# One inverse of a head's row sums, for all six query tiles, in place of two for three tiles each

## The chip, the cores and the metric

The kernel runs on one core of a Trainium2 chip. The metric is the device time of one execution in microseconds. The work is one program for five engines: TensorE (PE, with its weight loads PEld), VectorE (DVE), ScalarE (ACT), GpSimd (POOL) and SyncE (SP), which meet only through semaphores.

## What is computed

A masked attention, a mixture of experts with one expert per token, and a dense layer with a rational activation, one after the other. The change touches the attention alone:

```python
scores = scale * np.matmul(q, k.transpose(0, 1, 3, 2))
scores = np.where(mask, scores, -1000000000.0)     # mask: query and key have the same nearest centroid
scores = scores - np.max(scores, axis=-1, keepdims=True)
attn = np.exp(scores)
attn = attn / (np.sum(attn, axis=-1, keepdims=True) + 1e-09)
return np.matmul(attn, v)
```

There are 2 x 8 = 16 heads of 768 queries and keys, 64 wide. What is changed is how the divisor `sum + 1e-09` is inverted.

## The kernel before

A head has six tiles of 128 queries, in two groups of three. The heads run in `steps`, a routine that each engine has of its own, with six steps i = 0 to 5 a head; heads 0, 1 and 14, 15 are written out, heads 2 to 13 run in a hardware loop of two heads a turn. In step i, PE transposes the probabilities of tile i (L387) into two PSUM banks, computes the scores of tile i + 2 (L347, L348; in steps 4 and 5 these are tiles 0 and 1 of the next head), and does a piece of other work: products with the values (L362, L363), the transpose back of a group's outputs (`back`, L371), and the preparation of the next heads (L321, L329, L334). ACT splits the transposed probabilities (L675, tile PTH) and computes the exponentials of tile i + 1 (L644), whose sums it leaves in SM. DVE takes the rest of the split (L1023, PTL), in steps 0 and 1 the one-hot rows of the next head (L972 to L980), and the row maximum of tile i + 2 (L962). POOL makes the operands of the head after (L837, L852, L854), the split values (L864, L866) and the mask rows (L872, L875), and in eight of the heads one piece of a weight (L834).

The chain that closes a step is: maximum (DVE), exponential (ACT), transposes (PE), split (ACT, then DVE). PE may transpose tile i + 1 into a bank only when DVE has taken tile i out of it, and only when that tile's exponential is there.

`inverse_sums` (two DVE instructions, L989 and L991) makes the inverses of three row sums in RS, a tile of three columns; `normalise` (L997) multiplies a group's outputs in PSUM by them and writes them to XO, and PE may fill the output bank again (`values`, part 0, L359) only when that is done. In the order of DVE's instructions, the inverses of a head's first group are made at the end of step 4 and used at the start of the next head's step 0; those of its second group are made at the end of the next head's step 1 and used at the end of its step 2. Below, "the boundary" of a head is the stretch from the row maximum of its step 5 to the first split of the next head's step 0. Behind an odd head of the loop DVE's sequencer also goes through the loop's branch there (L1056).

Of the kernel before, what the change touches and what calls it, by code (L numbers as in the profile page):

```python
# [6 lines left out]
ALU = mybir.AluOpType  # L7
# [3 lines left out]
P = 128  # L11
B, H, S, D = 2, 8, 768, 64
C = 16
HEADS = B * H
HP = HEADS // 2
JT = S // P
# [10 lines left out]
GT = 3  # L27
HG = JT // GT
# [16 lines left out]
def needed(v):  # L45

    return not (isinstance(v, int) and v <= 0)


def program(nc, q, k, v, cent, emb, tau, w1, w2, w_in, w_out, coef_a, coef_b, cst, tokid, out, dbg=None):  # L50
# [4 lines left out]
    with ExitStack() as ctx:  # L55
# [3 lines left out]
        def sem(name):  # L59
            return ctx.enter_context(nc.semaphore(name))  # L60
# [31 lines left out]
        def esb(name, shape, dt=F32):  # L92
            return early.enter_context(nc.sbuf_tensor(name, shape, dt))
# [21 lines left out]
        OS = esb("OS", [P, GT * P])  # L115
        NM = esb("NM", [P, 2, JT])
        SM = esb("SM", [P, 2, JT])
        RS = esb("RS", [P, GT])
        AMX, AM2 = esb("AMX", [P, 2 * JT]), esb("AM2", [P, 2 * JT])
        AEQ = esb("AEQ", [P, 2 * JT, C])  # L120
        OH = esb("OH", [P, JT, P], BF16)
# [43 lines left out]
        max_done, exp_done, pth_done, ptl_done = (sem(n) for n in ("max_done", "exp_done", "pth_done", "ptl_done"))  # L165
        os_done, rs_done, xo_done = sem("os_done"), sem("rs_done"), sem("xo_done")
# [764 lines left out]
        def _(dve):  # L931
# [28 lines left out]
            def rowmax(g, par, i):  # L960
                dve.wait_ge(s_done, JT * g + i + 1)
                nc.vector.tensor_reduce(NM[:, par, i:i + 1], s_bank(i % 2), AX.X, ALU.max, negate=True).then_inc(max_done, 1)  # L962

            def one_hots(g, n):

                dots = prep[:, 0:2 * JT * C].rearrange("p (a c) -> p a c", c=C)
                wide = [P, 2 * JT, C]
                if n:
                    dve.wait_ge(arg_step, 4 * g + n)
                if n == 0:  # L970
                    dve.wait_ge(prep_pe, PREPS * g + 4)
                    nc.vector.tensor_reduce(AMX[:, :], dots, AX.X, ALU.max).then_inc(arg_step, 1)  # L972
                elif n == 1:
                    nc.vector.tensor_tensor(AEQ[:, :, :], dots, AMX[:, :].unsqueeze(2).to_broadcast(wide), ALU.is_ge).then_inc(arg_step, 1)
                elif n == 2:
                    nc.vector.tensor_tensor(AEQ[:, :, :], AEQ[:, :, :], desc16.unsqueeze(1).to_broadcast(wide), ALU.mult).then_inc(arg_step, 1)
                elif n == 3:
                    nc.vector.tensor_reduce(AM2[:, :], AEQ[:, :, :], AX.X, ALU.max).then_inc(arg_step, 1)
                else:
                    nc.vector.tensor_tensor(OH[:, :, 0:4 * C].rearrange("p j (w c) -> p j w c", w=2)[:, :, :, 0:C],  # L980
                                            AEQ[:, :, :].rearrange("p (j w) c -> p j w c", w=2),
                                            AM2[:, :].unsqueeze(2).to_broadcast(wide).rearrange("p (j w) c -> p j w c", w=2),
                                            ALU.is_equal).then_inc(onehot_done, 1)

            def inverse_sums(g, par, grp):

                y = HG * g + grp
                dve.wait_ge(exp_done, GT * (y + 1))
                nc.vector.tensor_scalar(RS[:, :], SM[:, par, GT * grp:GT * (grp + 1)], 1e-9, None, ALU.add).then_inc(rs_done, 1)  # L989
                dve.wait_ge(rs_done, 2 * y + 1)  # L990
                nc.vector.reciprocal(RS[:, :], RS[:, :]).then_inc(rs_done, 1)  # L991

            def normalise(g, grp):
                y = HG * g + grp
                dve.wait_ge(rs_done, 2 * y + 2)
                dve.wait_ge(back_done, y + 1)
                nc.vector.tensor_tensor(XO[:, bass.ds(JT * (g // H) + GT * grp, GT), bass.ds(D * (g % H), D)],  # L997
                                        obank[:, 0:GT * D].rearrange("p (j d) -> p j d", d=D),
                                        RS[:, :].unsqueeze(2).to_broadcast([P, GT, D]), ALU.mult).then_inc(xo_done, 1)

            def early_logits(t):
                dve.wait_ge(lg_done, t + 1)
                nc.vector.tensor_copy(LG0[:, t, :], prep[:, 0:E]).then_inc(lg0_done, 1)

            def low_piece(w, par, p):
                dve.wait_ge(w_high, 8 * w + p + 1)
                nc.vector.tensor_tensor(LOW[par][:, p, :], RAW[par][:, p, :], HIGH[par][:, p, :].bitcast(F32), ALU.subtract).then_inc(w_low, 1)  # L1007

            def steps(h0, start=False, end=False):
                for par in range(2):  # L1010
                    for i in range(JT):
                        h = h0 + par
                        n = JT * h + i
                        far = end and par == 1
                        before = not (start and par == 0)
                        if i == 0:
                            if before:
                                normalise(h - 1, 0)
                        for hf in range(2):

                            dve.wait_ge(pth_done, 2 * n + 1 + hf)
                            at = (i % GT) * P
                            nc.vector.tensor_tensor(PTL[i // GT][:, 3 * hf:3 * hf + 3, at:at + P],  # L1023
                                                    pt_bank[hf].rearrange("p (a q) -> p a q", a=3),
                                                    PTH[i // GT][:, 3 * hf:3 * hf + 3, at:at + P].bitcast(F32), ALU.subtract).then_inc(ptl_done, 1)
                            if far and i and hf == 0:
                                early_logits(i - 1)
                        if i < 2 and not far:
                            for m in ((0, 1), (2, 3, 4))[i]:
                                one_hots(h + 1, m)  # L1030
                        if i < 4:
                            rowmax(h, par, i + 2)
                        elif not far:
                            rowmax(h + 1, 1 - par, i - 4)
                        if before and i == 1:
                            inverse_sums(h - 1, 1 - par, 1)
                        if before and i == 2:
                            normalise(h - 1, 1)
                        if i == 4:
                            inverse_sums(h, par, 0)  # L1040
                        if end and par == 0 and i < 4:

                            low_piece(0, 0, i)
# [9 lines left out]
            dve.wait_ge(pro_pe, 2)  # L1053
            nc.vector.tensor_copy(eT[:, :, :], obank[:, 0:KD * E].rearrange("p (a b) -> p a b", a=KD)).then_inc(pro_dve, 1)
            steps(0, start=True)
            with dve.Fori(1, HP - 1) as pr:  # L1056
                steps(2 * pr)
            steps(HEADS - 2, end=True)
            normalise(HEADS - 1, 0)
            early_logits(JT - 1)  # L1060
            inverse_sums(HEADS - 1, 1, 1)
            normalise(HEADS - 1, 1)
            if dbg is not None:
                return
# [200 lines left out]
```

## Time and profile before

| | before |
|---|---|
| median of 3 runs | 836.32 us (833.25 to 838.16) |
| the profiled execution | 837.4 us, its span 835.5 us |
| PE, PEld, DVE, ACT, POOL busy | 93%, 86%, 73%, 55%, 42% of the span |
| attention | from about 20 to 306 us of the span |
| L989, L991, L997 | 32 instructions each |
| granted TensorE clock | 0.956 over the span, 1.00 in the heads of the loop |

The span is what the profiler saw between the first and the last instruction. A line of a timeline gives the start of an instruction and its duration in us, its engine, its line in the kernel, what it writes and reads, and in brackets how long the engine had been idle before it and who ended that. On DVE the recorded start of an instruction overlaps the end of the one before by some 0.08 us when the two follow one another without a gap. A line of `DVEq` is work of DVE's sequencer: arithmetic on registers for semaphore values and addresses, branches, and waits.

### The profile page before, as it was taken

What the parts mean: (1) busy time and instruction counts of PE and PEld (TensorE: products, weight loads), DVE (VectorE), ACT (ScalarE), POOL (GpSimd) and SP (SyncE); (2) the same over time, 40 slices, a digit from 0 to 9 for tenths busy, and PEclk for the clock granted to TensorE, in tenths of its full rate; (3) what the DMA queues carried; (4) which work ended last, traced back from release to release, by engine and by line L of the source; (5) the groups of instructions that cost most, each with busy time, mean ns of one, the idle gap of its engine ahead of it and who ended that gap; (6) DMA issues with size and microseconds to landing.
All of it is one profiled execution on the core that took longest, in us unless ns stands there. A gap on an engine that the chain in (4) does not pass through costs nothing.

```text
span 835.5 us, 15711 instructions
## 1 busy us (share of the span) xinstructions
PE 773.8 (93%) x5429; PEld 721.2 (86%) x5430; DVE 613.5 (73%) x986; ACT 458.5 (55%) x867; POOL 354.2 (42%) x334
## 2 busy tenths in 40 slices
PE   7999999999998993299999999989999999999996
PEld 4898999999997883199999999988989999999995
DVE  4688888888889736156666667679987787778773
ACT  4677777778777752011111111137777776766762
POOL 3666667665665003605324455543232232313232
PEclk9799999999999985599999999989999999999998
DMA  9311111111100024416655456650000000000000
GB/s 268 75 29 31 38 47 29 28 38 44 32 35 1 1 95 170 140 27 227 209 187 171 164 177 223 201 202 1 1 11 16 1 26 2 25 0 25 0 26 26
DMA packets 67908, 63.61 MB, mean 76 GB/s; under 512 B 30872, under 2 KB 53528, under 8 KB 67872
## 3 DMA queue, kind: packets, MB, share of 16 engines
q1 hardware_dynamic: 65024, 56.62, 21.5%
q0 software_dynamic: 1920, 6.30, 2.0%
q8 instruction: 20, 0.33, 0.2%
q10 hardware_dynamic: 928, 0.23, 0.1%
q14 instruction: 16, 0.13, 0.0%
HBM read 56.32 MB, written 6.82 MB: 76 GB/s over the span
## 4 chain that ended last, share of the span: by engine, by line
PE 51%; issue 23%; DVE 13%; POOL 8%; ACT 2%; DMA 1%; POOLq 0%; DVEq 0%; ACTq 0%
PE PS L519 8%; PE PS L520 8%; PE PS L521 8%; PE PS L387 6%; POOL HL L910 5%; PE PS L362 3%; PE PS L363 3%; PE PS L347 3%; PE PS L348 3%; PE PS L329 3%; DVE NM L962 2%; DVE PTL L1023 1%; DVE w_low L1007 1%; POOL out L919 1%; PE PS L371 1%
## 5 line engine op out<-in xcount | busy, mean ns | idle before, releaser
L519 PE MATMUL PS<-XH,w_high 128*128 128x256 f32 x640 | 183.5, 287 | 7.6 <-DVE XL L1190 3.6
L520 PE MATMUL PS<-XL,w_high 128*128 128x256 f32 x640 | 183.0, 286 | 0.0
L521 PE MATMUL PS<-XH,w_low 128*128 128x256 f32 x640 | 182.9, 286 | 0.0
L834 POOL TENSOR_SCALAR w_high<-w_raw 128x1024 fp32r<-128x1024 f32 x80 | 102.4, 1300 | 129.2 <-DMA w_raw<-in_moe_w 103.7
L910 POOL TENSOR_TENSOR HL<-U,HH 128x512 fp32r<-128x512 f32 x48 | 62.5, 1301 | 185.9 <-ACT HH L773 185.9
L519 PEld LDWEIGHTS PS<-XH,w_high 128*128 128x128 f32 x640 | 124.8, 195 | 10.5 <-issue 8.8
L1023 DVE TENSOR_TENSOR PTL<-PS,PTH 128x384 fp32r<-128x384 f32 x192 | 98.3, 551 | 40.4 <-ACT PTH L675 40.3
L520 PEld LDWEIGHTS PS<-XL,w_high 128*128 128x128 f32 x640 | 124.8, 195 | 1.7
L521 PEld LDWEIGHTS PS<-XH,w_low 128*128 128x128 f32 x640 | 124.7, 195 | 0.0
L1007 DVE TENSOR_TENSOR w_low<-w_raw,w_high 128x1024 fp32r<-128x1024 f32 x80 | 115.1, 1465 | 9.4 <-issue 9.4
L675 ACT ACTIVATE PTH<-PS 128x384 fp32r<-128x384 f32 x192 | 85.1, 490 | 47.9 <-PE PS L387 47.3
L962 DVE TENSOR_REDUCE NM<-PS 128x1 f32<-128x768 f32 x96 | 90.9, 947 | 3.9 <-PE PS L348 3.9
L387 PE MATMUL PS<-consts,PR 128*128 128x128 f32 x576 | 85.0, 283 | 8.5 <-DVE PTL L1023 7.2
L644 ACT ACTIVATE PR<-PS,NM 128x768 f32<-128x768 f32 x96 | 86.9, 905 | 5.5 <-DVE NM L962 5.5
L752 ACT ACTIVATE HH<-PS 128x512 fp32r<-128x512 f32 x32 | 19.1, 597 | 118.1 <-PE PS L521 118.1
L387 PEld LDWEIGHTS PS<-consts,PR 128*128 128x128 f32 x576 | 68.3, 147 | 16.9 <-DVE PTL L1023 7.6
L519 PE MATMUL PS<-w_high,HH 128*128 128x512 f32 x192 | 75.6, 394 | 3.3 <-POOL HL L910 1.7
L347 PE MATMUL PS<-B,A 128*128 128x512 f32 x192 | 74.7, 389 | 0.8 <-POOL A L875 0.8
L520 PE MATMUL PS<-w_low,HH 128*128 128x512 f32 x192 | 75.3, 392 | 0.0
L521 PE MATMUL PS<-w_high,HL 128*128 128x512 f32 x192 | 74.7, 389 | 0.0
L519 PE MATMUL PS<-HH,w_high 128*128 128x256 f32 x256 | 73.1, 286 | 0.0
L520 PE MATMUL PS<-HL,w_high 128*128 128x256 f32 x256 | 72.4, 283 | 0.0
(178 smaller groups left out, 1742.0 us busy)
## 6 DMA issues: line engine op xcount, KB each, us to landing
w_raw<-in_moe_w SPq DMA_DIRECT2D x64, 512.0 KB, 8.0
xs<-xs_dram SPq DMA_DIRECT2D x9, 513.0 KB, 3.6
w_raw<-in_moe_w_in SPq DMA_DIRECT2D x8, 512.0 KB, 8.1
w_raw<-in_moe_w_out SPq DMA_DIRECT2D x8, 512.0 KB, 7.2
QK<-in_q SPq DMA_DIRECT2D x16, 192.0 KB, 3.1
V<-in_v SPq DMA_DIRECT2D x16, 192.0 KB, 2.4
QK<-in_k SPq DMA_DIRECT2D x15, 192.0 KB, 3.2
xs_dram<-zeros SPq DMA_DIRECT2D x1, 513.0 KB, 4.0
```

Of the source, the lines that this page charges most:

```text
L347: nc.tensor.matmul(o[:, lo:hi], A1[par][:, cols], B1[par][:, lo:hi], start=True, stop=False)
L387: last = nc.tensor.transpose(pt_bank[hf][:, j * P:(j + 1) * P], PR[i % 2][:, c:c + P], ident)
L519: nc.tensor.matmul(o, wh, xh, start=first, stop=False)
L520: nc.tensor.matmul(o, wh, xl, start=False, stop=False)
L521: return nc.tensor.matmul(o, wl, xh, start=False, stop=last)
L644: nc.scalar.activation(PR[i % 2][:, :], s_bank(i % 2), ACT.Exp, bias=NM[:, par, i:i + 1], accum_out=SM[:, par, i:i + 1]).then_inc(exp_done, 1)
L675: nc.scalar.activation(PTH[grp][:, 3 * hf:3 * hf + 3, at:at + P], pt_bank[hf].rearrange("p (a q) -> p a q", a=3), ACT.Copy).then_inc(pth_d ...
L834: return nc.gpsimd.tensor_scalar(HIGH[par][:, p, :], RAW[par][:, p, :], 1.0, 0.0, ALU.mult, ALU.add)
L910: nc.gpsimd.tensor_tensor(HL[:, g:g + 2, :].rearrange("p a t -> p (a t)"), U[j % 2][:, :], HH[:, g:g + 2, :].rearrange("p a t -> p (a t)") ...
L962: nc.vector.tensor_reduce(NM[:, par, i:i + 1], s_bank(i % 2), AX.X, ALU.max, negate=True).then_inc(max_done, 1)
L1007: nc.vector.tensor_tensor(LOW[par][:, p, :], RAW[par][:, p, :], HIGH[par][:, p, :].bitcast(F32), ALU.subtract).then_inc(w_low, 1)
L1023: nc.vector.tensor_tensor(PTL[i // GT][:, 3 * hf:3 * hf + 3, at:at + P], pt_bank[hf].rearrange("p (a q) -> p a q", a=3), PTH[i // GT][:, 3 ...
```

## The change

RS gets six columns. `inverse_sums` works on all six sums of a head at once and stands at the end of step 5, in every head. It waits for the head's sixth exponential, and, from head 1 on, for the two `normalise` of the head before, since RS is written again. The two old calls (end of step 4, end of step 1 of the next head) and the one behind the last step are gone. `normalise` takes its three columns of RS and waits for the new count of `rs_done`. There are 16 pairs of L989 and L991 in place of 32.

```diff
-        RS = esb("RS", [P, GT])
+        RS = esb("RS", [P, JT])
...
-            def inverse_sums(g, par, grp):
-
-                y = HG * g + grp
-                dve.wait_ge(exp_done, GT * (y + 1))
-                nc.vector.tensor_scalar(RS[:, :], SM[:, par, GT * grp:GT * (grp + 1)], 1e-9, None, ALU.add).then_inc(rs_done, 1)
-                dve.wait_ge(rs_done, 2 * y + 1)
+            def inverse_sums(g, par):
+
+                dve.wait_ge(exp_done, JT * (g + 1))
+                if needed(g):
+
+                    dve.wait_ge(xo_done, HG * g)
+                nc.vector.tensor_scalar(RS[:, :], SM[:, par, :], 1e-9, None, ALU.add).then_inc(rs_done, 1)
+                dve.wait_ge(rs_done, 2 * g + 1)
                 nc.vector.reciprocal(RS[:, :], RS[:, :]).then_inc(rs_done, 1)
 
             def normalise(g, grp):
                 y = HG * g + grp
-                dve.wait_ge(rs_done, 2 * y + 2)
+                dve.wait_ge(rs_done, 2 * g + 2)
                 dve.wait_ge(back_done, y + 1)
...
-                                        RS[:, :].unsqueeze(2).to_broadcast([P, GT, D]), ALU.mult).then_inc(xo_done, 1)
+                                        RS[:, GT * grp:GT * (grp + 1)].unsqueeze(2).to_broadcast([P, GT, D]), ALU.mult).then_inc(xo_done, 1)
...
-                        if before and i == 1:
-                            inverse_sums(h - 1, 1 - par, 1)
                         if before and i == 2:
                             normalise(h - 1, 1)
-                        if i == 4:
-                            inverse_sums(h, par, 0)
+                        if i == 5:
+                            inverse_sums(h, par)
...
             early_logits(JT - 1)
-            inverse_sums(HEADS - 1, 1, 1)
             normalise(HEADS - 1, 1)
```

## Rows read from the trace of the kernel before

**Rows 1.** Busy time in one head: stretch and length, each engine's, then granted clock, DMA

```profile
116.19:133.00 16.81, 16.48 (x123) 15.35 (x122) 14.41 (x29) 13.11 (x30) 11.51 (x13) 1.00 0.15 35
```

**Rows 2.** Waits of PE's weight loads in 60 to 252 us: total, times, longest

```profile
PEld PS L387 <- DVE PTL L1023: 7.6, 23, 0.6
```

**Rows 3.** Chain of waits in one head, in order of time: start, length, what

```profile
115.54 0.62 DVE RS L989
...
116.30 0.57 DVE PTL L1023
```

**Rows 4.** All instructions of L989: duration in ns, least, median, most

```profile
L989 DVE TENSOR_SCALAR RS<-SM x32: 151/158/798, 38.7 to 305.1; 128x3 f32<-128x3 f32 x32
```

**Rows 5.** Timeline of POOL

```profile
29.32 0.51 POOL L864 TENSOR_SCALAR VS<-V 128x384 fp32r<-128x384 f32 x1
...
115.13 1.00 POOL L866 TENSOR_TENSOR VS<-V,VS 128x384 fp32r<-128x384 f32 x1
...
125.47 0.83 POOL L837 TENSOR_SCALAR A<-T 64x768 fp32r<-64x768 f32 x1
...
131.13 0.73 POOL L864 TENSOR_SCALAR VS<-V 128x384 fp32r<-128x384 f32 x1 [1.02 <-PE PS L363]
```

**Rows 6.** Timeline of DVE: the second pair of a head, and head 14's L989

```profile
115.46 0.70 DVE L989 TENSOR_SCALAR RS<-SM 128x3 f32<-128x3 f32 x1
116.19 0.18 DVE L991 RECIPROCAL RS<-RS 128x3 f32<-128x3 f32 x1
...
269.09 0.16 DVE L989 TENSOR_SCALAR RS<-SM 128x3 f32<-128x3 f32 x1
```

**Rows 7.** Timeline of DVE: two instructions that start together with one of POOL's

```profile
29.38 0.66 DVE L976 TENSOR_TENSOR AEQ<-AEQ,consts 128x192 f32<-128x192 f32 x1
...
131.13 0.36 DVE L980 TENSOR_TENSOR OH<-AEQ,AM 128x192 bf16<-128x192 f32 x1
```

**Rows 8.** Timeline of DVE: step 5 of head 5, the boundary, head 6

```profile
123.72 1.02 DVE L1023 TENSOR_TENSOR PTL<-PS,PTH 128x384 fp32r<-128x384 f32 x2 [0.64 <-ACT PTH L675]
124.66 0.95 DVE L962 TENSOR_REDUCE NM<-PS 128x1 f32<-128x768 f32 x1
125.53 0.35 DVE L997 TENSOR_TENSOR XO<-PS,RS 128x192 f32 x1
126.32 1.02 DVE L1023 TENSOR_TENSOR PTL<-PS,PTH 128x384 fp32r<-128x384 f32 x2 [0.45 <-ACT PTH L675]
127.43 0.36 DVE L972 TENSOR_REDUCE AMX<-PS 128x12 f32<-128x192 f32 x1
...
128.10 0.95 DVE L962 TENSOR_REDUCE NM<-PS 128x1 f32<-128x768 f32 x1
129.42 1.02 DVE L1023 TENSOR_TENSOR PTL<-PS,PTH 128x384 fp32r<-128x384 f32 x2 [0.37 <-ACT PTH L675]
...
301.31 0.36 DVE L997 TENSOR_TENSOR XO<-PS,RS 128x192 f32<-128x192 f32 x1 [0.16 <-PE PS L371]
```

**Rows 9.** Timeline of ACT: the last instruction of two exponentials

```profile
32.83 0.19 ACT L644 ACTIVATION_READ_ACCUMULATOR PR<-PS,NM 128x1 f32 x1
...
116.46 0.19 ACT L644 ACTIVATION_READ_ACCUMULATOR PR<-PS,NM 128x1 f32 x1
```

**Rows 10.** Timeline of PE's weight loads

```profile
33.68 0.19 PEld L347 LDWEIGHTS PS<-B,A 128*128 128x128 f32 x1
...
117.65 0.19 PEld L347 LDWEIGHTS PS<-B,A 128*128 128x128 f32 x1
...
127.20 0.19 PEld L362 LDWEIGHTS PS<-PTH,VS 128*128 128x128 f32 x1
...
301.78 0.19 PEld L362 LDWEIGHTS PS<-PTH,VS 128*128 128x128 f32 x1 [0.38 <-issue]
```

**Rows 11.** DVE's sequencer at the boundary of head 5: durations in ns, first and last start

```profile
L1056 DVEq ALU_OP  x1: 40/40/40, 124.2 to 124.2; - x1
...
L997 DVEq FUSED_REGOPS  x2: 46/154/263, 124.8 to 125.1; - x2
```

## The prediction

> **What bounds the kernel now.** I read the page first, then the attention alone, since nothing else is touched. Busy time in one head of the loop [rows 1]: the head takes 16.81 us and PE is busy for 16.48 of them at a granted clock of 1.00 (the 2.4 GHz level), so PE sets the pace and only its gaps can be won. The waits say which gaps [rows 2]: in eleven and a half heads, PE's weight loads waited 7.6 us in 23 waits, all for PTL, the split on DVE; that is two waits a head. The chain of waits places them [rows 3]: DVE's L989, 0.62 us of it on the path, then the split of step 2 at 116.30, whose end releases PE's transposes of step 3. So of a head's two pairs, the second one (end of step 1) lies on the path. The first (end of step 4) does not: DVE waits 0.64 us for ACT behind it, at 123.72 [rows 8].
>
> Why is one of the two long? L989 has a median of 158 ns and a maximum of 798 [rows 4]. The one of 0.70 us starts at 115.46 [rows 6] while POOL's L866 runs from 115.13 to 116.13 [rows 5], and ends at 116.16, 0.03 behind it; the other twelve of this kind are the same picture. In head 14, where POOL's instruction had ended, the same L989 takes 0.16 us [rows 6]. So it is held by a running POOL instruction. The Trainium skill, SBUF — State Buffer, "Who interferes with whom", says that the two engines share a port pair that a VectorE instruction of this kind needs for itself, that the one that issues first keeps it for its whole instruction, and that two-input instructions of VectorE are caught too; the trace agrees with all of it, here and in the two starts of [rows 7].
>
> **What the removal gives.** Without the pair at the end of step 1, the split of step 2 starts right behind the row maximum, 0.84 us earlier (116.30 less 115.46). That is not what PE gains: what is late next is tile 3's exponential, which ends at 116.46 + 0.19 = 116.65 [rows 9]. In head 0 such an exponential is the last to come: from its end, 32.83 + 0.19 = 33.02, to the weight load of L347 at 33.68 [rows 10] it is 0.66 us. Head 0 is written out; in the loop I add an estimated 0.06 for a register instruction behind the wait. So L347's load comes at 116.65 + 0.72 = 117.37 in place of 117.65 [rows 10]: **0.28 us a head**, for heads 1 to 13. The bounds are 0.34 (no register instruction) and 0.20 (twice that). In head 14 the pair is short, and 0.16 + 0.18 and its gaps less the overlap, 0.28, come off a path that ends in a split of the weights and PTL; gain 0.28. The first pair (step 4) stands before the 0.64 us of waiting, the one behind the last step before a wait for PE's `back`: nothing.
>
> **What the new place costs.** At the end of step 5 the new L989 starts 0.87 behind the row maximum's start, where L997 starts now: 125.53 [rows 8]. POOL is then in the fourth of its four L837, from 125.47 to 126.30 [rows 5]; this L837 starts 0.03 to 0.06 us before in all 14 heads that have it. Who gets the port? When both start within a hundredth (131.13 [rows 5, 7]), DVE goes first: L980 takes its usual 0.36, and L864 0.73 instead of 0.51. When POOL is 0.06 ahead (29.32 against 29.38 [rows 5, 7]), DVE is held: L976 ends at 30.04, 0.21 behind POOL's end, instead of taking 0.35. The 0.05 of the new place is nearer to the second row, so I take it that **the new L989 is held to 126.33**. The bounds are 0.16 us (won) and 0.80 (held). By the rule of the Trainium skill cited above, the first to issue keeps the pair, which would be L837, and the sum would be the forecast's; read as a rule on who starts moving data first, it would leave the tie open and allow rival 1.
>
> A second cost has no row. `normalise` comes right behind now. Today its sequencer work (address arithmetic, behind its wait for `rs_done`) runs while the row maximum is busy: two register instructions of 0.26 and 0.05 us, from 124.8 to 125.18 [rows 11]. With the wait for a reciprocal that has only just been issued, they come after it, in the open. Reciprocal 126.36 to 126.56 (0.18 for three columns [rows 6], 0.20 taken for six; at most twice 0.18). Then:
> - behind an even head: 0.03 for the semaphore, 0.34 for the register instructions, 0.05 to issue: L997 starts at 126.98 in place of 125.53, ends at 127.33.
> - behind an odd head the loop's branch stands there too. From L1056 at 124.2 to the end of L997's register work at 125.18 it is 0.98 us [rows 11], some 0.03 of it the issue of the row maximum; the 0.95 left starts when the reciprocal is issued (126.36): L997 starts at 127.36, ends at 127.71.
> - behind head 0 everything is written out and has no register work: L997 at 126.60.
>
> Lower bound of this cost: nothing, if the register work is ahead of the wait.
>
> PE needs L997 for L362, whose weights it loads at 127.20 [rows 10]. From L997's end to this load it is 0.11 in the one row where it is the last to come (301.31 + 0.36 to 301.78 [rows 8, 10]), and about 0.04 where the wait sits on the load itself, as behind odd heads. So PE is late by 127.33 + 0.11 - 127.20 = 0.24 (even) and 127.71 + 0.04 - 127.20 = 0.55 (odd); behind head 0 by nothing.
>
> DVE itself: two splits, 0.94 from start to what follows; L972 to the row maximum 0.67; row maximum to split 0.87 [rows 8]. Even: split at 127.25, L972 at 128.19, maximum at 128.86, split of step 1 at 129.73, and 1.71 on L980 at 131.44. Odd: the same 0.38 later, 131.82. POOL's L864 is released by PE: 131.13 + 0.24 = 131.37 (even), 131.13 + 0.55 = 131.68 (odd). So **the tie at 131.13 is broken**: POOL is ahead by 0.07 and 0.14. L980 is then held to L864's end plus 0.21: 131.88 + 0.21 = 132.09 and 132.19 + 0.21 = 132.40, in place of 131.49, late by 0.60 and 0.91. The maximum, the exponential and the transposes of step 3 hang on L980; the 0.28 comes off. Net: **0.32 slower a head behind an even one, 0.63 behind an odd one**.
>
> The added wait for `xo_done` is for a `normalise` three steps back; behind it on DVE stand L989, L991 and L997, and it costs one sequencer instruction, hidden behind the row maximum. The wait for the sixth exponential is met before step 5 (its transposes need it). No DMA is moved. The columns that L989 and the reciprocal have more are in the numbers above. In the last head, new L989, reciprocal and L997 follow one another with L997 waited for by PE (301.31 [rows 8]): 0.19 later.
>
> **The sum**, in the profiled execution: 6 even boundaries of the loop (behind heads 2 to 12) at +0.32 = +1.9; 6 odd (1 to 11) at +0.63 = +3.8; behind head 0 -0.28; head 14 -0.28; the last head +0.19. Together +5.3 us, 837.4 to 842.7. The profiled execution is 1.1 us over the median of the runs, so for the median 836.3 + 5.3 = **841.6 us**.
>
> **Rivals.**
> 1. *The port is won.* The new L989 is issued before POOL holds the pair and takes 0.16; L997 then starts at 126.33 (even) or 126.72 (odd), which the waits of DVE behind it cover (0.45 us before 126.32, 0.1 before 127.43, 0.37 before 129.42, and the overlaps of 0.08 [rows 8]; behind odd heads only just), and PE is not kept. Then only the gain is left: 13 x -0.28 - 0.28 + 0.19 = -3.8, 832.5 us. The same comes out if L989 is held but the register work runs ahead of the wait. For it: the threshold lies anywhere between 0.00 and 0.06, and behind head 1 the distance is only 0.03. Against it: the row at 0.06, and 0.05 is close to it. The Trainium skill, VectorE: DVE Perf Modes, "Rules for kernel authors", advises fewer instructions for chained ones ("Minimize op *count*, not sems"), and there are 32 fewer; that speaks for this side.
> 2. *Only the first tie is lost.* Behind even heads L980 is just 0.07 behind by a chain of five terms. If it still goes first, it is late by 131.80 - 131.49 = 0.31, which the 0.28 cancels: 6 x 0.03 + 3.8 - 0.37 = +3.6, 839.9 us.
> 3. *POOL's next instruction follows without letting DVE in*, L852 of 1.8 us: L997 would be late by 1.8 more and PE with it, 12 x 1.8 = 22 us more. Against it: L989 got in right behind L866 thirteen times although L834 was queued. That the change does not do what it says I see no way for.
>
> **How the numbers follow.** L989 held at most boundaries: 0.68, of which the forecast (841.6) has 0.42 and rival 2 (839.9) 0.26. Rival 1 (832.5): 0.28, some of it with a mixture over the heads. Rival 3: 0.02. The rest, 0.02, is what I have not seen. A measurement of this kernel can tell about 0.5%, 4.2 us, from no change: under 832.1 is faster, over 840.5 slower. The forecast lies over that line by 1.1 (0.8 of its chance), rival 2 under it by 0.6 (0.25 of its), rival 1 is 0.4 short of the other line (0.4 of its). That gives faster 0.12, within 0.5% 0.46, slower 0.42. The range has to take in rival 1 above and the bounds of the chain: 831.8 to 843.6. The forecast's own range is 839.5 to 843.6.
>
> **What would show it.** L989 x16, at the end of step 5, of about 0.8 us in 14 heads or 0.16; L980 of about 0.8 us or 0.36; PE's L362 of step 0 waiting for L997; PE's wait for PTL in step 3 gone in favour of the exponential; a head of the loop 17.3 us long on average, or 16.5. The forecast is wrong if L989 is short, or if L997 starts within 0.1 us of the reciprocal's end.

## The result and the profile after

The changed kernel takes 840.14 us (median of 20 runs, 836.51 to 843.66) against 834.23 us of the kernel before beside it (20 runs, 832.02 to 838.17). The ratio over the runs timed side by side is 1.0058, interval 1.0042 to 1.0074: 4.8 us slower, where the forecast had 5.3. (The two medians by themselves are 5.9 us apart; in what follows "ratio" is always the first kind.) 64 instructions of DVE became 32, and the kernel is slower.

Its profiled execution took 843.66 us. The page's span and busy times:

```profile
span 841.6 us, 15646 instructions
...
PE 775.0 (92%) x5429; PEld 722.5 (86%) x5430; DVE 612.5 (73%) x954; ACT 458.3 (54%) x867; POOL 349.8 (42%) x334
```

Two heads of the loop by windows, columns as in [rows 1]; the first contains the boundary behind an odd head (5), the second the one behind an even head (6):

```profile
116.10:133.60 17.50, 16.54 (x123) 15.43 (x122) 14.51 (x28) 13.09 (x31) 11.29 (x13) 1.00 0.13 34
133.60:150.74 17.14, 16.47 (x123) 15.44 (x122) 14.52 (x28) 13.03 (x31) 11.27 (x13) 1.00 0.14 34
```

PE has no more work than in [rows 1] (16.5 us at a clock of 1.00) and more idle time. Each window also carries what the one-hots' L980 costs at its start, not at its end (L980 runs from 115.84 and from 133.36, see below). The instructions of the new pair and of `normalise`, as in [rows 4]: duration in ns (least, median, most), first and last start:

```profile
L991 DVE TENSOR_SCALAR RS<-SM x16: 159/816/827, 41.7 to 305.8; 128x6 f32<-128x6 f32 x16
...
L993 DVE RECIPROCAL RS<-RS x16: 190/191/192, 42.6 to 306.0; 128x6 f32<-128x6 f32 x16
...
L999 DVE TENSOR_TENSOR XO<-PS,RS x32: 339/357/359, 42.8 to 310.7; 128x192 f32 x24, 128x192 f32<-128x192 f32 x8
```

L991 (L989 before) is now long in 14 of 16 cases; before it was in 13 of 32. The last normalisation, which ends attention, starts at 310.7; before it is at 305.8, 4.9 sooner; the other 1.4 of the 6.3 us between the two profiled executions lie behind attention. Of the 4.9, 0.7 had come up before the first head, where nothing is changed. The rows of ACT's L636, which comes once a head, show where the rest is. The first pair is of before, the second of after, each the third and the fifteenth of these instructions:

```profile
49.30 0.79 ACT L636 ACTIVATE OHT<-PS 48x768 f32<-48x768 bf16 x1
...
251.14 0.79 ACT L636 ACTIVATE OHT<-PS 48x768 f32<-48x768 bf16 x1
```

```profile
49.46 0.79 ACT L636 ACTIVATE OHT<-PS 48x768 f32<-48x768 bf16 x1
...
256.27 0.79 ACT L636 ACTIVATE OHT<-PS 48x768 f32<-48x768 bf16 x1
```

Between them lie the twelve boundaries behind heads 1 to 12: 201.84 us before and 206.81 after, +5.0. These **twelve heads** are the measure of the mechanism in what follows, since the start of the kernel, the first head and the stage behind attention differ between the profiled executions also where nothing was changed in them.

The waits in 60 to 252 us, the stretch of [rows 2]:

```profile
DVE XO L999 <- DVE RS L993: 7.2, 12, 0.8
PEld PS L387 <- DVE PTL L1025: 6.9, 11, 0.7
ACT PR L644 <- DVE NM L962: 5.6, 11, 0.6
PE PS L387 <- ACT PR L644: 5.4, 11, 0.6
PEld PS L362 <- DVE XO L999: 2.8, 6, 0.6
```

The 23 waits of [rows 2] are 11: the one that the held pair of step 1 caused is gone. In its place step 3 waits for the exponential (5.4 us), and PE waits for `normalise` (2.8), which waits for the reciprocal (7.2).

DVE's timeline at an even boundary (head 4) and at an odd one (head 5), to be laid beside [rows 8]:

```profile
109.09 0.95 DVE L962 TENSOR_REDUCE NM<-PS 128x1 f32<-128x768 f32 x1
109.96 0.81 DVE L991 TENSOR_SCALAR RS<-SM 128x6 f32<-128x6 f32 x1
110.81 0.19 DVE L993 RECIPROCAL RS<-RS 128x6 f32<-128x6 f32 x1
111.42 0.36 DVE L999 TENSOR_TENSOR XO<-PS,RS 128x192 f32 x1 [0.42 <-DVE RS L993]
...
115.84 0.70 DVE L980 TENSOR_TENSOR OH<-AEQ,AM 128x192 bf16<-128x192 f32 x1
...
126.24 0.95 DVE L962 TENSOR_REDUCE NM<-PS 128x1 f32<-128x768 f32 x1
127.10 0.81 DVE L991 TENSOR_SCALAR RS<-SM 128x6 f32<-128x6 f32 x1
127.94 0.19 DVE L993 RECIPROCAL RS<-RS 128x6 f32<-128x6 f32 x1
128.94 0.36 DVE L999 TENSOR_TENSOR XO<-PS,RS 128x192 f32 x1 [0.80 <-DVE RS L993]
...
133.36 0.67 DVE L980 TENSOR_TENSOR OH<-AEQ,AM 128x192 bf16<-128x192 f32 x1
...
150.48 0.36 DVE L980 TENSOR_TENSOR OH<-AEQ,AM 128x192 bf16<-128x192 f32 x1
```

And POOL's instructions that start beside them:

```profile
109.92 0.82 POOL L837 TENSOR_SCALAR A<-T 64x768 fp32r<-64x768 f32 x1
...
115.83 0.51 POOL L864 TENSOR_SCALAR VS<-V 128x384 fp32r<-128x384 f32 x1 [1.28 <-PE PS L363]
...
150.47 0.73 POOL L864 TENSOR_SCALAR VS<-V 128x384 fp32r<-128x384 f32 x1 [1.29 <-PE PS L363]
```

Three things are to be seen. L991 ends at 110.77, 0.03 behind POOL's L837 (110.74), as L989 did behind L866 in [rows 5, 6]. Behind the reciprocal DVE sits idle with nothing to wait for, 0.42 and 0.80 us: the register work of `normalise`. And L980, 0.36 us in [rows 7], takes 0.70 at 115.84 and 0.67 at 133.36. At 150.48 it takes 0.36 and POOL's L864 0.73: there DVE got the port.

### The profile page after: what moved, and what is told of

Read it like the earlier page. It is cut to its first block, busy times and chain, and to the rows that moved or that the text cites. A ratio compares the mean times of both kernels' runs of the same rounds, so it can differ in the third digit from the quotient of the medians.

```text
span 841.6 us, 15646 instructions
## 1 busy us (share of the span) xinstructions
PE 775.0 (92%) x5429; PEld 722.5 (86%) x5430; DVE 612.5 (73%) x954; ACT 458.3 (54%) x867; POOL 349.8 (42%) x334
## 4 chain that ended last, share of the span: by engine, by line
PE 44%; issue 26%; DVE 17%; POOL 8%; ACT 3%; DMA 1%; DVEq 1%; POOLq 0%; ACTq 0%
PE PS L519 8%; PE PS L520 8%; PE PS L521 8%; POOL HL L910 5%; PE PS L387 4%; DVE NM L962 4%; DVE PTL L1025 3%; PE PS L362 3%; PE PS L363 3%; PE PS L347 2%; PE PS L348 2%; DVE w_low L1009 1%; POOL out L919 1%; PE PS L321 1%; DVE RS L991 1%
## 5 line engine op out<-in xcount | busy, mean ns | idle before, releaser
L834 POOL TENSOR_SCALAR w_high<-w_raw 128x1024 fp32r<-128x1024 f32 x80 | 100.2, 1272 | 133.9 <-DMA w_raw<-in_moe_w 109.3
```

What stands on the lines that cost most here:

```text
L834: return nc.gpsimd.tensor_scalar(HIGH[par][:, p, :], RAW[par][:, p, :], 1.0, 0.0, ALU.mult, ALU.add)
```

## The experiments

All were timed beside the kernel before, in five rounds each. The twelve heads are from the profiled execution of each, in us against the 201.84 of the kernel before.

### The port alone: x1

```diff
+        RT = esb("RT", [P, 3, 4])
...
-                nc.vector.tensor_scalar(RS[:, :], SM[:, par, :], 1e-9, None, ALU.add).then_inc(rs_done, 1)
+                nc.vector.tensor_scalar(RT[:, :, 0:2], SM[:, par, :].rearrange("p (a b) -> p a b", b=2), 1e-9, None, ALU.add).then_inc(rs_done, 1)
                 dve.wait_ge(rs_done, 2 * g + 1)
-                nc.vector.reciprocal(RS[:, :], RS[:, :]).then_inc(rs_done, 1)
+                nc.vector.reciprocal(RS[:, :].rearrange("p (a b) -> p a b", b=2), RT[:, :, 0:2]).then_inc(rs_done, 1)
```

Everything is where the change has it; only the shape of the addition's output differs, so that its outermost size is 3 where the input's is 6.

> The changed kernel, but the sums plus 1e-9 go to a tile of three pairs set 4 columns apart (the reciprocal reads them there). Theory (POOL's running L837 holds the added instruction because it needs the port pair; the Trainium skill, VectorE: DVE Perf Modes, What auto-detection actually checks, says the two-port mode wants the outermost sizes of source and destination both even or equal, here 6 and 3): the instruction takes under 0.3 us in all heads, L997's successor starts about 0.6 earlier, PE is not kept, L980 keeps its 0.36; the gain of 0.28 a head is left: ratio to the kernel before about 0.995 (-3.8 us). Rival (the hold is something else, such as the wait for the exponential or the new wait for xo_done): it stays at 0.8 us and the ratio at 1.006.

Measured: 832.56 us against 835.91, ratio 0.9954 (0.9928 to 0.998); twelve heads -3.2. The forecast's rival 1 has -0.28 a head, 3.4 in twelve, and 832.5 us in all. One of the twelve heads is 16.89 us long in place of 16.53: there L980 (L981 here) lost its tie with POOL and took 0.67 us. So the tie is close even where `normalise` keeps nobody. The timeline of DVE and POOL at a boundary:

```profile
107.51 0.15 DVE L992 TENSOR_SCALAR RT<-SM 128x6 f32<-128x6 f32 x1
107.70 0.19 DVE L994 RECIPROCAL RS<-RT 128x6 f32<-128x6 f32 x1
108.31 0.36 DVE L1000 TENSOR_TENSOR XO<-PS,RS 128x192 f32 x1 [0.42 <-DVE RS L994]
...
107.48 0.83 POOL L838 TENSOR_SCALAR A<-T 64x768 fp32r<-64x768 f32 x1
```

The addition starts 0.03 behind POOL as before, and takes 0.15 beside it. The register work is in the open as ever (0.42), and costs nothing. The Trainium skill, VectorE: DVE Perf Modes, "What auto-detection actually checks", says that an operation with a single source, both source and output in SBUF, takes the mode that uses the second port if their outermost sizes are both even or equal; 6 and 3 are neither, and the trace agrees.

### The same detour with equal sizes: y1

To see that it is the sizes and not the other tile or the strides, `SM` was laid out as `[P, 2, 3, 4]` too, which makes them 3 and 3.

```diff
-        SM = esb("SM", [P, 2, JT])
+        SM = esb("SM", [P, 2, 3, 4])
...
-                nc.vector.tensor_scalar(RT[:, :, 0:2], SM[:, par, :].rearrange("p (a b) -> p a b", b=2), 1e-9, None, ALU.add).then_inc(rs_done, 1)
+                nc.vector.tensor_scalar(RT[:, :, 0:2], SM[:, par, :, 0:2], 1e-9, None, ALU.add).then_inc(rs_done, 1)
```

> The changed kernel with the sums plus 1e-9 in three pairs set 4 columns apart, as in x1_oneport, but now the sums themselves lie in three pairs set 4 apart too, so that outermost sizes of source and destination are equal (3 and 3). Theory (x1_oneport was not held because its sizes, 6 and 3, rule out the form that needs the port pair): the instruction is held again, 0.8 us in 14 heads, and the ratio is back at 1.004 to 1.007. Rival (the other tile or its address was what freed it in x1_oneport): under 0.2 us and 0.995.

Measured: 841.05, ratio 1.0053 (1.0029 to 1.0078); twelve heads +4.6. The addition is held again:

```profile
L992 DVE TENSOR_SCALAR RT<-SM x16: 159/816/832, 41.4 to 304.9; 128x6 f32<-128x6 f32 x16
```

### The pair ahead of the row maximum: x2

```diff
+                        if i == 5:
+                            inverse_sums(h, par)
                         if i < 4:
...
-                        if i == 5:
-                            inverse_sums(h, par)
```

> The changed kernel, but in step 5 the inverses stand ahead of the row maximum instead of behind it. Theory (half of the cost is the register work of the normalise, exposed because it follows the reciprocal at once): the added instruction is still held, now by the third L837, by up to 0.8 us, but the register work runs under the row maximum and the normalise follows it without a gap; PE is not kept, or by under 0.1 us, and L980 is not held: ratio 0.994 to 0.998. Rival (the 0.8 us of the hold alone sets the loss, wherever it stands in step 5): 1.004 to 1.006.

Measured: 833.65, ratio 0.9971 (0.9947 to 0.9996); twelve heads -3.3. DVE's timeline:

```profile
106.35 0.80 DVE L991 TENSOR_SCALAR RS<-SM 128x6 f32<-128x6 f32 x1
107.18 0.19 DVE L993 RECIPROCAL RS<-RS 128x6 f32<-128x6 f32 x1
107.29 0.95 DVE L962 TENSOR_REDUCE NM<-PS 128x1 f32<-128x768 f32 x1
108.15 0.35 DVE L999 TENSOR_TENSOR XO<-PS,RS 128x192 f32 x1
```

The addition is held as long as in the kernel after (0.80), by the L837 before, but a row maximum of 0.95 us covers the register work again: `normalise` starts 0.86 behind the maximum with no idle time. So the hold alone costs nothing at this place, and by x1 the register work alone costs nothing. Only the two in a row (0.65 and 0.4 to 0.8 us) outrun the waits of DVE that used to cover them.

### The one-hots' tie undone: x3

```diff
                 pool.wait_ge(v_in[par], 16 * (g // 2) + 16)
+                pool.wait_ge(onehot_done, g + 1)
```

This stands ahead of L864: POOL can't start there before L980 has ended.

> The changed kernel, but POOL's L864 waits for L980 (the one-hot rows) to be done, so it can't hold it. Theory (two steps of the loss: PE and the splits late by 0.3 to 0.7 us, then L980 held by L864): L980 takes 0.36 in all heads, behind even heads nothing is lost (+0.03), behind odd heads 0.4 remains: 6 x 0.03 + 6 x 0.41 - 0.4 = +2.3 us, ratio 1.003. Rival (L980's hold is hidden by what PE waits for anyway): 1.006 as without the wait.

Measured: 836.47, ratio 1.0000 (0.9974 to 1.0025); twelve heads +2.2, 2.8 less than in the kernel after. L980 is never held (357 to 359 ns in all), L991 still is. Windows of a head behind an even and one behind an odd head:

```profile
99.12:115.96 16.84, 16.46 (x123) 15.42 (x123) 14.23 (x29) 13.05 (x29) 11.33 (x12) 1.00 0.14 35
115.96:133.17 17.21, 16.55 (x123) 15.41 (x122) 14.20 (x29) 13.18 (x29) 11.32 (x12) 1.00 0.14 34
```

The heads are as long as expected (+0.02 behind even ones, +0.31 to +0.47 behind odd ones of the loop, where 0.03 and 0.41 were expected; only behind head 1 it is +0.11). The total is not: 1.003 was expected, which lies just outside the interval. In the profiled execution the difference lies outside the twelve heads: from the first L636 to the last normalisation, attention is 0.2 us longer than before, so the ends of it gain 2.0, where 0.4 was expected. Why they do was not taken apart. The kernel after gives the same price by itself: the two heads behind even ones in which its L980 took 0.36 us are 16.80 long, and the four in which it was held 17.14. A lost tie costs about 0.3 us of a head.

### The kernel before without the addition: x4

```diff
-                nc.vector.tensor_scalar(RS[:, :], SM[:, par, GT * grp:GT * (grp + 1)], 1e-9, None, ALU.add).then_inc(rs_done, 1)
-                dve.wait_ge(rs_done, 2 * y + 1)
-                nc.vector.reciprocal(RS[:, :], RS[:, :]).then_inc(rs_done, 1)
+                nc.vector.reciprocal(RS[:, :], SM[:, par, GT * grp:GT * (grp + 1)]).then_inc(rs_done, 1)
```

> The kernel before, at its old places with its two calls a head, but without L989: the reciprocal reads the sums directly. It leaves out the addition of 1e-9. Theory (all that the change could win was the hold of L989 at the end of step 1, and what is late next is the exponential): the gap of the split of step 2 closes by 0.65 to 0.7 us, PE gains 0.28 a head: 14 x 0.28 = 3.9 us, ratio 0.995. Rival (the count of instructions is what matters, not the hold): 32 instructions fewer of 0.16 us, of which half on the path, 2.5 us, ratio 0.997; rival (the whole hold is on the path): 13 x 0.62 = 8 us, ratio 0.990.

Measured: 831.06, ratio 0.9956 (0.9931 to 0.9981); twelve heads -2.9, most heads 16.53 us in place of 16.82. The second reciprocal of a head starts while L866 runs, and all 32 are short:

```profile
L989 DVE RECIPROCAL RS<-SM x32: 157/165/168, 38.9 to 301.6; 128x3 f32<-128x3 f32 x32
```

So the gain of 0.28 a head that the forecast gave the removal comes from this one addition; the reciprocal, which stays, costs nothing. The ratio alone couldn't tell this from the rival of 0.997, the lengths of the heads do; that it is the addition's hold and not the addition itself is shown by x8, which keeps it. In two heads L980 lost its tie (0.71 us), and these are 16.89 long. And a RECIPROCAL is not held where a TENSOR_SCALAR of the same shape is.

### The kernel before, L864 behind L980: x8

The edit of x3, made to the kernel before.

> The kernel before, only with L864 behind L980. L864 then starts about 0.55 us later and L866 within a few hundredths of the L989 of step 1. Theory (who starts first holds): if L866 is ahead, L989 lasts 1.0 us in place of 0.70, a head 17.1 us, ratio 1.005; if L989 is ahead or level, it takes 0.16, a head 16.5 us, ratio 0.995. Rival (the port has no part in it): L989 stays at 0.70 and the ratio at 1.000.

Measured: 830.59, ratio 0.9938 (0.9915 to 0.9962); twelve heads -3.6. The wait was put there for the order of the one-hots, and moved POOL's next one as well:

```profile
113.83 0.16 DVE L990 TENSOR_SCALAR RS<-SM 128x3 f32<-128x3 f32 x1
...
113.89 1.00 POOL L867 TENSOR_TENSOR VS<-V,VS 128x384 fp32r<-128x384 f32 x1
```

DVE starts 0.06 ahead of POOL and isn't held; POOL's instruction keeps its 1.00 us too. One wait on another engine gives all that the removal of a pair gives.

### A freer order, with the change and without: x5, x6, x7, y2

The runs so far leave PE a gap of 0.2 us a head (x1: busy for 16.34 of 16.54) and step 3 waiting for the split and the exponential. x5 has the change with the additions of x1, the place of x2, the wait of x3, and two moves in the order:

```diff
                         elif i == 2:
-                            if not far:
-                                prep_part(h + 1, 1 - par, 4)
                             if before:
                                 back(h - 1, 1)
+                            if not far:
+                                prep_part(h + 1, 1 - par, 4)
...
-                        if i < 2 and not far:
-                            for m in ((0, 1), (2, 3, 4))[i]:
+                        if i == 0 and not far:
+                            for m in (0, 1):
                                 one_hots(h + 1, m)
...
                             rowmax(h + 1, 1 - par, i - 4)
+                        if i == 1 and not far:
+                            for m in (2, 3, 4):
+                                one_hots(h + 1, m)
```

In step 1 the row maximum, on which an exponential hangs, goes ahead of the one-hots, and in step 2 PE does `back`, for which DVE waits, ahead of the one-hots' transposes.

> The changed kernel with all its collisions taken out and step 1 to 3 reordered: the sums plus 1e-9 in three pairs (no hold), inverses ahead of the row maximum in step 5, row maximum ahead of the one-hot rows in step 1, PE's transpose back ahead of the one-hot transposes in step 2, and L864 behind L980. Theory (what was late next behind the removed pair is the exponential of tile 3, so an earlier row maximum frees PE down to its own work): PE's transposes of step 3 follow the transpose back without a gap, a head of the loop 16.1 to 16.2 us in place of 16.82: 14 x 0.65 = 9 us, ratio 0.989 to 0.990. Rival (ACT becomes the bound, since the copy of the one-hot rows now stands late before its split): 16.4 to 16.5 us a head, ratio 0.994 to 0.995.

Measured: 823.30 us (822.34 to 825.85), ratio 0.9848 (0.9817 to 0.9878); twelve heads -7.0: the fastest version here, 1.5% under the kernel before. A head by windows, and PE's waits in 60 to 252 us:

```profile
110.67:126.85 16.18, 16.18 (x123) 15.24 (x121) 13.80 (x28) 12.89 (x30) 11.34 (x12) 1.00 0.15 36
...
PEld PS L388 <- issue: 1.3, 8, 0.2
```

PE is busy for the whole head at a clock of 1.00. The line of waits is the largest of PE's and of its weight loads; neither the split nor the exponential is among them. In the heads of the loop nothing is left to win from DVE. The heads are as expected (16.1 to 16.2 us), but the ratio is below the expected 0.989 to 0.990, and its interval leaves that out: in the profiled execution a shorter start and a shorter stage behind attention come on top, of which more below.

x6 is x5 without the wait ahead of L864.

> The same without L864 waiting for L980. Theory: the one-hot instructions stand one row maximum later and meet L864 and L866 of POOL, both are held, by some 0.4 and 0.5 us; the split of step 2 comes behind them: a head 16.5 to 16.6 us, ratio 0.995 to 0.997, so the order alone gives nothing over a free port. Rival (holds of the one-hot rows do not matter once the row maximum is ahead of them): as with the wait, 0.990.

Measured: 832.13, ratio 0.9944 (0.9922 to 0.9966); twelve heads -3.5. In DVE's and POOL's timelines two instructions of the one-hots are held in turn, one by each of POOL's:

```profile
113.42 0.64 DVE L977 TENSOR_TENSOR AEQ<-AEQ,consts 128x192 f32<-128x192 f32 x1
114.10 0.35 DVE L979 TENSOR_REDUCE AM<-AEQ 128x12 f32<-128x192 f32 x1
114.49 0.68 DVE L981 TENSOR_TENSOR OH<-AEQ,AM 128x192 bf16<-128x192 f32 x1
...
113.35 0.51 POOL L865 TENSOR_SCALAR VS<-V 128x384 fp32r<-128x384 f32 x1 [1.00 <-PE PS L364]
113.95 1.00 POOL L867 TENSOR_TENSOR VS<-V,VS 128x384 fp32r<-128x384 f32 x1
```

That one wait is worth half of what x5 gains in the twelve heads, and 8.8 us between the medians. An order on DVE is worth what POOL leaves of it.

x7 is the kernel before with x5's order and wait, and both old pairs.

> The kernel before with both its pairs of inverses at their old places, and only the reordering: row maximum ahead of the one-hot rows in step 1, transpose back ahead of the one-hot transposes in step 2, L864 behind L980. Theory: L989 of step 1 now starts some 0.2 us ahead of L864 and is not held (0.16 us); two short instructions on the path of 0.3 us are all that is left, 16.2 to 16.4 us a head, ratio 0.990 to 0.993, so most of the gain needs no change of the inverses. Rival (L989 is still held by POOL): over 16.7 us, ratio 0.998 or more.

Measured: 830.13, ratio 0.9925 (0.9895 to 0.9955); twelve heads -6.3, its additions never held (153/159/164 ns). So the new order and the wait together bring 6.3 of the 7.0 (the wait alone 3.6, x8), and the change, where no pair is held any more, 0.06 us a head. The medians of x5 and x7 are 6.8 us apart all the same, from six runs each. The profiled executions, the fastest of each, are 4.6 apart; 1.4 of that lie before the first head and 1.1 in the first (its L636 starts at 14.59 in x5 and 15.94 in x7, the next one at 30.33 and 32.75); what makes the start shorter I haven't taken apart, and it isn't put down to the change.

y2 is x5 with the plain additions of the change.

> As x5_free_slot, but with the plain inverses of the changed kernel (same tile, no pairs), ahead of the row maximum in step 5. Theory: the first instruction is held there for up to 0.8 us by an L837 as in x2_ahead, and since the normalise behind it has its register work under the row maximum, nothing of it reaches PE: 16.2 us a head, ratio 0.985 to 0.989, as x5_free_slot. Rival (with PE's slack gone the hold shows): 16.4 us a head or more, 0.990 or more.

Measured: 824.91, ratio 0.9870 (0.9842 to 0.9898); twelve heads -7.0 as in x5, though its addition is held (median 770 ns). So in the freer order the shape of x1 isn't needed: the hold is hidden, as in x2.

## Why the prediction was right

The forecast was followed from the row maximum of step 5 on. Its times behind that instruction's start (124.66 in [rows 8]), and those of the kernel after (109.09 and 126.24 in the rows above):

| behind the row maximum's start, us | even, forecast | even, after | odd, forecast | odd, after |
|---|---|---|---|---|
| addition starts | 0.87 | 0.87 | 0.87 | 0.86 |
| `normalise` starts | 2.32 | 2.33 | 2.70 | 2.70 |
| PE's load of L362 | 2.78 | 2.80 | 3.09 | 3.11 |
| POOL's L864 starts | 6.71 | 6.74 | 7.02 | 7.07 |
| L980 starts | 6.78 | 6.75 | 7.16 | 7.12 |
| L980 ends | 7.43 | 7.45 | 7.74 | 7.79 |

The rows of PE's weight loads behind the third line, and POOL's L864 of the odd boundary:

```profile
111.89 0.19 PEld L362 LDWEIGHTS PS<-PTH,VS 128*128 128x128 f32 x1 [0.17 <-issue]
...
129.35 0.19 PEld L362 LDWEIGHTS PS<-PTH,VS 128*128 128x128 f32 x1 [0.49 <-DVE XO L999]
...
133.31 0.51 POOL L864 TENSOR_SCALAR VS<-V 128x384 fp32r<-128x384 f32 x1 [1.64 <-PE PS L363]
```

Point by point:

- **The gain of 0.28 a head.** Right. x1, x2, x4 and x8 have it by four ways, with most heads 16.53 us long in place of 16.82. What is late next is the exponential, as was said: x1's PE waits for it 2.9 us in 12 waits.
- **The addition is held to POOL's end.** Right, and it decides the sign: x1 changes this alone and gets rival 1's time. The additions start 0.03 to 0.04 us behind POOL's L837, closer than the 0.05 of the forecast, and all 14 lose.
- **The register work in the open.** Right in both sizes, though no row of before had it; only behind head 1, from which the loop is entered, it is 0.57 us in place of 0.80. It is a cost only together with the hold (x1 and x2). The forecast added the two without saying that each alone would be hidden; rival 1 had that for one of them.
- **The tie with L864 is lost.** Right for odd boundaries. For even ones the forecast had POOL 0.07 ahead at the end of a chain of five terms, and it is 0.01: four were lost and two won, one of these at 150.48 as a tie and one because L864 came 0.27 late. Rival 2 was true of two heads in six. The mis-sized terms are small, 0.03 each: POOL starts 0.03 later, L980 0.03 sooner. That the four were lost is in part luck: L980 started 12 to 17 ns behind POOL there, and ties of up to 4 ns are won.
- **The sum.** Forecast against measured, from one L636 to the next: behind head 0 -0.28 against -0.40; six even boundaries +1.9 against +1.3 (the two ties won); six odd ones +3.8 against +3.7 (five at +0.59 to +0.70 and the one behind head 1 at +0.37, where the forecast had +0.63); head 14 -0.28 against -0.30; the last head +0.19 against +0.05. That is 5.3 against 4.3. By the ratio the kernels differ by 4.8, with an interval of 3.5 to 6.2 that holds both.
- **The chances.** By the ratio the kernel is 0.58% over the kernel before, just beyond the line between "within 0.5%" and "slower"; its median of 840.1 us is just under the 840.5 at which the forecast drew that line. That both had close to half was the right reading.

Rival 3 didn't come: in all 14 boundaries the addition got in between the fourth L837 and L852. Two slips in the forecast's working changed nothing. Its argument against this rival counts thirteen heads with L834 queued behind L866, but L834 stands there in eight of them. And the lower bound of the gain, with twice the register instruction, comes out at 0.22 a head and not 0.20.

## What to carry to other kernels

Of two short instructions on one engine, the place decides and not their number: look in the trace at what the other engine of the port pair is doing at the new place's time, and at which instruction used to cover the register work of the next one. Keep a long instruction between a small result and its user on the same engine, so that the sequencer's work behind the wait runs beside it. Where two engines start within hundredths of a microsecond of each other every time round, one wait that fixes their order can be worth more than the work removed (x8, and x5 against x6).

## What the runs showed of the hardware

**Who gets the port is decided by a few nanoseconds.** L980 and L864 start together in many heads of many of these kernels. In the start times of the traces, which go to the nanosecond, L980 kept its usual 0.36 us when it started up to 4 ns behind L864, and was held when it started 5 ns or more behind (5 ns twice in x4, 6 ns in x2, 12 to 92 ns in the others). The lost and the won case of the kernel after (115.84 against 115.83, and 150.48 against 150.47) look the same in hundredths. The Trainium skill, SBUF — State Buffer, "Who interferes with whom", says that who issues first keeps the pair; the traces agree but for these 4 ns, in which L980 won although it started second. The difference is too small to plan with: an order that matters has to be made by a wait.

**A shape can free an addition from the port.** 0.82 us beside POOL with sizes 6 and 6 (the kernel after) or 3 and 3 (y1), 0.15 with 6 and 3 (x1). For so small an operation nothing is lost: with POOL idle the plain one takes 0.16.

**The clock falls behind attention, at a varying place.** Windows of the kernel before, and of x5, behind the end of attention (columns as in [rows 1]):

```profile
305.00:310.00 5.00, 4.23 (x31) 3.85 (x31) 2.15 (x9) 3.31 (x9) 0.00 (x0) 0.87 0.54 178
...
308.00:309.00 1.00, 1.00 (x10) 1.00 (x10) 0.09 (x1) 0.82 (x4) 0.00 (x0) 0.86 1.06 367
```

```profile
300.00:305.00 5.00, 3.27 (x30) 3.09 (x28) 2.47 (x10) 3.99 (x6) 0.00 (x0) 0.97 1.07 371
305.00:310.00 5.00, 0.34 (x2) 0.13 (x2) 4.32 (x18) 0.28 (x1) 0.00 (x0) 0.50 0.53 196
```

In the kernel before attention ends at 306.1; the granted clock is 1.00 until 308, 0.86 in the next microsecond and 0.50, the 1.2 GHz level, from 309 on, while PE is still busy. In x5 attention ends at 294.6, and the clock reaches 0.50 only at 305, when all but two of PE's instructions of this stage are done. From the start of the last normalisation to the first multiplication by the gate it takes 15.8 us in x5 and y2, 19.6 before, 19.8 after, and between 16.0 (x7) and 20.5 (x4) in the others, with 74 instructions on PE in it in every one. The later the clock falls behind attention's end, the shorter the stage, to within 0.2 us and in all twelve profiled executions: about 10 us behind in x5, x7 and y2 (15.8 to 16.0 us), 6 in x8 (16.4), 4 in x1 and x2 (18.1 and 17.9), 1 to 3 in the other six (19.6 to 20.5). So 3.8 us of what x5 gains in its profiled execution come from there. Whether the scatter of single executions (832.0 to 838.2 us for the kernel before) comes from it too is not shown. The place doesn't go simply with the time at which attention ends (x4 and x8 start the last normalisation at 302.3 and 301.7 and take 20.5 and 16.4 us from there); what sets it stays open.
